# Attention part of a three-stage kernel: who issues and who computes the decay work, and the order of the score products

## The reference, cut to what matters

```python
def _attn_ref(q, k, v, lam):            # q, k, v: (2, 8, 768, 64); lam: one decay rate for each head
    for b in range(nb):                 # blocks along the sequence
        intra = einsum('bhic,bhjc->bhij', qb, kb) * Dmask      # scores, times lam**(i-j) for i >= j
        intra = einsum('bhij,bhjd->bhid', intra, vb)
        inter = einsum('bhid,bhde->bhie', qb * lam_pow, kv_state)
        out[:, :, sl] = intra + inter
        kb_dec = kb * rev_pow                                  # keys, times lam**(block-1-j)
        kv_state = lam_block * kv_state + einsum('bhsd,bhse->bhde', kb_dec, vb)

x = silu(attn @ w_gate) * (attn @ w_val) @ w_out               # MLP, 1536 tokens, 512 -> 1536 -> 512
out = gate_prob * (relu(x @ w1[e]) @ w2[e])                    # e: the expert that the token chose
```

## Time and profile before

| | |
|---|---|
| median of 3 runs | 535.24 us (535.2 to 535.6) |
| the profiled execution | 536.05 us, its span 534.3 us |
| busy share of the span | PE 98%, DVE 66%, ACT 46%, POOL 14% |
| instructions | 8608 |
| attention part | about the first 48 us |
| DMA, whole span | 84.57 MB, mean 158 GB/s |

### The profile page before, as it was taken

One profiled execution on the slowest core, in us unless ns is written; L12 is line 12 of the kernel. 1 busy time (PEld: TensorE's weight loads), 2 busy tenths in 40 slices (PEclk: granted clock), 3 DMA queues, 4 the chain that ended last, 5 costly groups with the idle time before them and its releaser, 6 DMA issues.

```text
span 534.3 us, 8608 instructions
## 1 busy us (share of the span) xinstructions
PE 525.4 (98%) x3275; PEld 447.9 (84%) x3275; DVE 353.3 (66%) x609; ACT 247.1 (46%) x414; POOL 74.4 (14%) x94
## 2 busy tenths in 40 slices
PE   8999999999999999999999999999999999999995
PEld 7998888888888887887888888778999999999994
DVE  7889898796775647644556666567667666766620
ACT  4325464635354425442434544465555565555511
POOL 4991000000000000010000020023021130311001
PEclk9999999999999999999999999999999999999999
DMA  8997304213030305645244666267575656654001
GB/s 291 339 302 255 137 21 158 104 54 126 32 120 20 119 0 176 187 158 230 81 138 133 203 196 237 81 212 238 210 272 204 206 221 215 220 201 169 1 28 36
DMA packets 22281, 84.57 MB, mean 158 GB/s; under 512 B 3804, under 2 KB 3804, under 8 KB 18656
## 3 DMA queue, kind: packets, MB, share of 16 engines
q1 hardware_dynamic: 17376, 71.35, 39.0%
q0 software_dynamic: 3712, 10.54, 5.6%
q10 hardware_dynamic: 1152, 2.13, 1.0%
HBM read 75.59 MB, written 10.53 MB: 161 GB/s over the span
## 4 chain that ended last, share of the span: by engine, by line
PE 95%; issue 2%; DVE 1%; POOL 1%; POOLq 0%; ACT 0%
PE bank L934 18%; PE bank L859 16%; PE bank L1161 15%; PE bank L1171 12%; PE bank L867 12%; PE bank L891 6%; PE bank L1075 2%; PE bank L1094 2%; PE bank L783 2%; PE bank L821 1%; PE bank L794 1%; PE bank L1150 1%; PE bank L829 1%; PE bank L961 1%; PE bank L1204 1%
## 5 line engine op out<-in xcount | busy, mean ns | idle before, releaser
L1609 DVE TENSOR_TENSOR ewl<-stages,ewh 128x1024 fp32r<-128x1024 f32 x50 | 60.8, 1223 | 16.9 <-ACT ewh L1248 16.6
L1248 ACT ACTIVATE ewh<-stages 128x1024 fp32r<-128x1024 f32 x50 | 52.2, 1054 | 0.7 <-DMA stages<-expert_w 0.7
L1554 ACT ACTIVATE ehh<-bank 128x256 fp32r<-128x256 f32 x48 | 18.5, 385 | 58.1 <-PE bank L1161 58.0
L636 POOL DMA_DIRECT2D stages<-expert_w x8 | 4.6, 572 | 260.9 <-DVE more_hl L1609 185.3
L1171 PE MATMUL bank<-ewl,ehh 128*128 128x512 f32 x96 | 37.8, 394 | 0.0
L1171 PE MATMUL bank<-ewh,ehl 128*128 128x512 f32 x96 | 37.7, 393 | 0.0
L1171 PE MATMUL bank<-ewh,ehh 128*128 128x512 f32 x96 | 37.5, 391 | 0.0
L1161 PEld LDWEIGHTS bank<-exh,ewh 128*128 128x128 f32 x224 | 33.2, 188 | 3.6
L1161 PE MATMUL bank<-exh,ewh 128*128 128x256 f32 x224 | 36.0, 283 | 0.0
L2092 DVE SCALAR_TENSOR_TENSOR ehl<-bank,ehh 128x256 fp32r<-128x256 f32 x48 | 20.2, 422 | 23.8 <-ACT ehh L1554 23.7
L1161 PE MATMUL bank<-exl,ewh 128*128 128x256 f32 x224 | 34.9, 278 | 0.0
(11 more groups left out here) (291 smaller groups left out, 1248.6 us busy)
## 6 DMA issues: line engine op xcount, KB each, us to landing
stages<-expert_w SPq DMA_DIRECT2D x21, 1024.0 KB, 4.9
stages<-mlp_w SPq DMA_DIRECT2D x24, 768.0 KB, 4.5
stages<-attn_in SPq DMA_DIRECT2D x18, 512.0 KB, 5.6
stage<-expert_w SPq DMA_DIRECT2D x7, 1024.0 KB
stages<-expert_w POOLq DMA_DIRECT2D x8, 512.0 KB, 5.7
stage<-attn_in SPq DMA_DIRECT2D x6, 512.0 KB, 5.8
held<-c SPq DMA_DIRECT2D x12, 256.0 KB, 2.0
stages<-held SPq DMA_DIRECT2D x12, 256.0 KB, 2.8
```

Source lines behind the costliest of these rows:

```text
L1248: return nc.scalar.activation(dst, src, ACT.Copy)
L1554: nc.scalar.activation(ehh[f % 2][:, :], bank[:, H_BANK + f % 2, 0:CAP], ACT.Relu).then_inc(ehh_ready, 1)
L1609: V.tensor_tensor(dst, src, high.bitcast(F32), ALU.subtract).then_inc(inc, 1)
```

## The change

The decay rates are issued from ACT's own queue, as ACT's first instruction, in place of SP's; the router's weights are issued by SP behind the last tile of the attention. POOL takes `queries(n)` ahead of `keys(n)`. The fading of the state goes from POOL (one instruction) to ACT (four, one for each pair of heads), where it follows `attention_tile(n-2)`. From n = 5 on, PE takes the scores of two tiles in a row in every odd tile and none in the even ones. DVE takes the first `add_state(0)` behind `weigh(1)`, and the `turn`s at tiles 8, 9, 11 and 11 in place of 8, 9, 10 and 11.

```diff
@@ constants
+PAIRED = 5
@@ block.sync
-            sp.dma_start(lam_sb[:, :], lam_rows).then_inc(lam_landed, 16)
             for s in range(4):
                 attention_in(s, s)
-                if s == 0:
-                    sp.dma_start(router[:, :, 0:E], router_w).then_inc(router_landed, 16)
             for n in range(4, NT):
                 sp.wait_ge(o_ready, n - 3)
                 attention_in(n % 4, n)
+            sp.dma_start(router[:, :, 0:E], router_w).then_inc(router_landed, 16)
@@ block.gpsimd
-            def fade(n):
-                pool.wait_ge(state_ready, 2 * (n - 1))
-                nc.gpsimd.tensor_tensor(faded[n % 2][:, :, :], state[n % 2][:, :, :],
-                                        powers[:, H:H + NPAIR, P:P + 1].broadcast_to([P, NPAIR, P]),
-                                        ALU.mult).then_inc(faded_ready, 1)
-
             for n in range(1, NT):
+                if n >= 2:
+                    queries(n)
                 if n < LAST_STATE:
                     keys(n)
-                if n >= 2:
-                    queries(n)
-                if 2 <= n < LAST_STATE:
-                    fade(n)
@@ block.tensor
                 if 1 <= n < LAST_STATE:
                     to_state(n)
-                if 1 <= n < NT - 1:
-                    scores(n + 1)
+                for m in (n + 1,) if 1 <= n < PAIRED else (n + 1, n + 2) if n >= PAIRED and n % 2 else ():
+                    if m < NT:
+                        scores(m)
                 within(n)
@@ block.scalar
+            act.dma_start(lam_sb[:, :], lam_rows).then_inc(lam_landed, 16)
             act.wait_ge(powers_step, 12)
...
+            act.wait_ge(pair_step, 8)
+
+            def fade(n):
+                act.wait_ge(state_ready, 2 * (n - 1))
+                for a in range(NPAIR):
+                    last = nc.scalar.activation(faded[n % 2][:, a, :], state[n % 2][:, a, :], ACT.Copy,
+                                                scale=powers[:, H + a, P:P + 1])
+                last.then_inc(faded_ready, 1)
+
             for n in range(NT):
                 attention_tile(n)
+                if n + 2 < LAST_STATE:
+                    fade(n + 2)
@@ block.vector
                 weigh(n)
                 if n == NT - 1:
                     split_gate_val(0, 0)
+                if n == 1:
+                    add_state(0)
                 if n >= 1:
                     tokens_low(n - 1)
-                if n < LAST_STATE:
+                if 1 <= n < LAST_STATE:
                     add_state(n)
-                if n >= NT - 4:
-                    turn(1, n - (NT - 4))
+                for t in {NT - 4: (0,), NT - 3: (1,), NT - 1: (2, 3)}.get(n, ()):
+                    turn(1, t)
```

## The result

The changed kernel takes 539.37 us (median of 6 runs, 538.43 to 542.02), the kernel before, run beside it, 535.47 (535.2 to 536.3). The ratio is 1.0079, with a 95% interval of 1.0055 to 1.0103. The forecast was 534.5 us, with a range of 533.6 to 536.0: wrong in sign and outside the range. The profiled execution has 540.78 us, its span 538.9; it is the second longest of the six, so what its trace shows is more than the median lost (4.73 us against 3.90).

A forecast was written before the change was run, and what follows sets the result against it. PE bounds the kernel (95% of the span), so reaching the MLP earlier counts: -1.45 at the MLP, +0.15 and +0.1 for turns, +0.5 for decay rates, -0.7 us from 535.24, giving 534.5 us, range 533.6 to 536.0.

The forecast's parts named there:

- The decay rates: At the start: issued from ACT's queue beside tile 0 they land later, 0.5 us covered, loss 0.5 us.
- x: How much later the decay rates land at the start: between 0 and 3.3 us, taken as 1.0.
- rival 1: At tile 0's to_state and the table chain: decay rates very late, 3.3 us, total 536.8 us; chance 0.13.
- Tile 0 earlier: At the start: tile 0 issued 0.46 us earlier, its scores up to 0.2 us earlier, gain 0.1 us.
- Queries first: On POOL: queries ahead of keys end tile 2's from_state wait of 0.50 us; with the earlier start, gain 0.6.
- Fades on ACT at 0: Each tile's state fade on ACT, 1.28 us, fits beside its copies and nothing waits: value 0.
- The pairs: Scores of two tiles in a row on PE: seams give 0.3 us, tile 9's wait eats part, 0.15 left.
- rival 2: Paired scores of tiles 9 and 11 wait for their tiles, landing at 5.6 us: total 536.0 us; chance 0.08.
- The router at 0: Router's weights, 16 KB ahead of the MLP's first weights, which have 0.3 us to spare: cost 0.
- The tail: Before the MLP: DVE's chain decides from tile 7's within, one turn fewer ahead of gvl, MLP at 46.9 us.
- rival 4: Tail reorderings do nothing, as PE or the first weights hold the MLP up: 535.1 us; chance 0.08.
- rival 3: In the tail a DVE turn falls whole behind POOL's queries, costing up to 1.06 us: 535.4 us; chance 0.09.

The follow-up runs named there:

- e2: Kernel before with one edit, the decay rates issued first from ACT's queue instead of SP's: 538.22 us, ratio 1.0035.
- e3: Changed kernel with 16 dummy products in place of 3 in PE's wait ahead of tile 0's to_state: 537.87 us, ratio 1.0030.
- e4: Kernel before with decay rates on ACT's queue and SP's transfers held until they landed: 536.75 us (one execution); the rates landed after 1.6 us.
- e1: Changed kernel, but SP issues the decay rates first again, as before: 537.05 us, ratio 1.0020.
- e6: Changed kernel with decay rates by SP first and the router's weights behind the first six transfers of MLP weights, pairs kept: 536.47 us, ratio 1.0016.
- e11: Kernel before with queries ahead of keys and the router's weights behind the first six transfers of MLP weights: 536.01 us, ratio 1.0000.
- e7: Kernel before with one edit, POOL takes queries ahead of keys: 535.11 us, ratio 0.9987.
- e9: Kernel before with queries ahead of keys and the fades on ACT: 535.13 us, ratio 0.9982.
- e13: Changed kernel with decay rates and router's weights both issued by SP where they were before: 536.24 us, ratio 1.0012.
- e5: Changed kernel with decay rates by SP first and without the pairs, router at its new place: 536.98 us, ratio 1.0018.
- e8: Changed kernel with decay rates by SP first, no pairs, and the router's weights behind the first six transfers of MLP weights: 535.78 us, ratio 1.0002.
- e10: Kernel before with queries ahead of keys and the turns at tiles 8, 9, 11 and 11: 535.48 us, ratio 0.9985.
- e15: Kernel before with queries ahead of keys, fades on ACT and the last two turns behind DVE's first sigmoid product: 535.11 us, ratio 0.9991.

## Why the prediction was wrong, by its steps

- **The decay rates: the step that failed.** The forecast took x = 1.0 and a loss of 0.5 us. x was 3.3 (5.89 less 2.57), the upper end that it had named; in e2 and e3, with the rates and tile 0 issued in the same way, it was 2.5. The cover was 0.6 (3.32 less 2.71), about the 0.5 that was said. The reason for halving, "at the start SP's traffic only begins", is wrong: tile 0 was issued in the same instant, and the rates' pieces went between its pieces. The row of the router (5.0 us) was the nearest after all, and rival 1 the right case for this term, though its 536.8 us was too low. The Trainium skill ("DMA: Bandwidth & Descriptors", Queues, rings and completion order) has the engines take turns between the queues, and that spoke against the change; e2 and e4 bear it out (4.2 us beside tile 0, 1.6 alone). Only the turns look shorter here than the 9 to 17 descriptors it names: summed over the engines, 107 pieces of the one beside 122 of the other in 2 us, and the last ones still behind 4.5 us.
- **The clock: a term that was missing.** Even rival 1 counted only the wait. A wait of 1.8 to 2.9 us on PE ahead of T(0) put it at the lower clock until 16 to 19 us, another 1.6 (e2) to 2.7 us (e3 against the change). This holds for the profiled executions. The mean granted clock of the changed kernel's six is 0.993 (the profiled one) and 0.991 (542.02 us), but 0.997 to 1.000 in the other four, no lower than in the kernel before; and that with 1.000, which has no room for such a fall, still took 539.47 us. So the clock is not shown to be the whole of the 2.6 us between rival 1's 536.8 and 539.4. The rest of the change is there too: rival 1 counted it as a gain of 1.2 us, and e1 has it as a loss of 1.2. How the two share the difference stays open.
- **Tile 0 earlier: not in every run.** Issued 0.46 us earlier it landed 4.9 us after issue in place of 4.3, at about 5.7 both times; in e2 and e3, issued at the same moment, it landed after 4.1 and 4.0 us, at 4.9. The 0.1 us of gain was nothing in the changed kernel, and where PE idles for tile 0 the rise to the full rate can be later (e6, e11).
- **Queries first: right.** F(2) 0.50 us earlier (e7), and 0.84 at the MLP.
- **Fades on ACT at 0: right** (e9).
- **The pairs: wrong in sign where the start is not late.** The seams gave more than assumed: S to S in one row took 1.99 us, 0.2 less than two, and two tiles with a pair took 6.56 us (F(6) to F(8)) in place of 6.91, 0.35 a pair where the forecast had 0.15. But the tiles' landing was taken from the best rows (4.8). Where PE waited most it was 5.2 to 6.2 us, and S(7), S(9), S(11) waited by 0.2 to 1.7 (e1, e3, e13): rival 2, which had 0.08. In the changed kernel itself the tiles on which the pairs wait landed after 4 us. There it took 32.57 us from F(2) to the MLP where the forecast had 32.5, but that is luck: W(7) came 20.34 us behind F(2) in place of 20.8, and the MLP 12.2 behind W(7) in place of 11.7, since gvl waited for the first weights.
- **The router at 0: wrong.** Ahead of the first weights it may cost 0.16% when no pairs are in the way (e5 against e8), but the intervals overlap, and the weights landed after 6.8 us in both. Its absence behind tile 0 costs 0.1 to 0.2% (e11 against e10 and e9).
- **The tail.** The DVE chain was read rightly (xl(7) to weigh(11) took 7.56 us in place of 7.44), but the 0.3 us that the first weights had to spare was all there was: with the turns moved gvl waits for them (rival 4; 0.29 us in the changed kernel, where they landed after 6.4 us). The turn of tile 9 did not meet `queries(11)`: it took 0.69 us, and the 0.15 for it, like rival 3, did not come.

The sum of the parts: the rates by ACT cost 0.35% (e2) to about 0.6% (e1 against the change), the rest of the change 0.2% (e1). In that rest queries first gains 0.15%, the pairs cost 0.2 to 0.3% (e13 against e15 and e9), and the router's place 0.1 to 0.2% (e11), overlapping.

## What to carry to other kernels

A small transfer on which the whole start hangs goes out first and alone; issued at the same time as bulk loads from another queue it lands with them, not ahead of them. Price a wait on the matrix engine with the clock that it loses, not only with its length, and where the wait can't be avoided fill it with dummy products, but no more than the wait holds. When transfers run near their limit, an earlier use of their data turns straight into a wait, and one profile may not show it.

## What the runs showed of the hardware

- Two hardware queues that started together were served side by side, about one for one summed over the transfer engines: 107 pieces of 48 bytes beside 122 of 4 KB in 2 us.
- The granted clock fell to 0.50 after 1.8 us without products (e2), and stayed there to about 16.3 us, in the change to about 19.2 (from the mean clock of the stretch from 15 to 20 us: 0.87 and 0.58, between 0.50 and 1.00).
- At the start the granted clock reads 1.00 while products still take double time (e11: 2.04 us for four dummies, x8 in the rows, 1.16 in e9), so there it has to be read from the durations.
